# Two vector instructions moved ahead of three others in the first group of three MLP blocks

## The reference

```
xn = (x - mu) / sqrt(var + 1e-6) * g_ln
ch = max(xn @ w_ch1, 0) @ w_ch2        # 512 -> 2048 -> 512, 4 x 576 rows
x  = x + ch
```

## Time and profile before

| | |
|---|---|
| median of 3 runs | 932.4 us (932.03 to 933.45) |
| profiled execution | 932.03 us, span 930.2 us |
| PE busy / PEld busy | 908.8 us (98%) / 841.2 us (90%) |
| DVE / ACT / POOL busy | 707.1 us (76%) / 545.5 us (59%) / 552.2 us (59%) |
| first MLP, blocks 2, 3, 4 | about 444.5 to 710 us of the span |
| group 0 of blocks 2, 3, 4 | second products from 452.7, 539.2 and 625.9 us |

### The profile page before, as it was taken

The page is one execution under the profiler, slowest core; times in us unless marked ns, Lnnn a source line. Parts: engine busy times, 40 slices in busy tenths (PEclk is TensorE's granted clock), DMA queues, the critical chain, the costliest instruction groups (busy, mean ns, idle before and its releaser), DMA issues.

```text
span 930.2 us, 18185 instructions
## 1 busy us (share of the span) xinstructions
PE 908.8 (98%) x6153; PEld 841.2 (90%) x6153; DVE 707.1 (76%) x1155; ACT 545.5 (59%) x1184; POOL 552.2 (59%) x547
## 2 busy tenths in 40 slices
PE   4999999999999999999999999999999999999998
PEld 3999999999989999999899988898988989989897
DVE  4899989989998899942767878789998672663623
ACT  3899999999989666543655655565565221212110
POOL 4989889898873477665566668758986210010100
PEclk9999999999999999999999999999999999999999
DMA  6243233234213233100000000002200001010011
GB/s 179 65 104 93 68 94 100 66 90 103 69 41 110 71 95 122 35 1 1 1 1 1 1 1 1 1 3 68 91 25 1 1 1 46 1 50 8 1 47 57
DMA packets 44874, 44.46 MB, mean 48 GB/s; under 512 B 14017, under 2 KB 34753, under 8 KB 44673
## 3 DMA queue, kind: packets, MB, share of 16 engines
q1 hardware_dynamic: 44368, 43.21, 16.8%
q10 hardware_dynamic: 432, 0.30, 0.1%
HBM read 28.81 MB, written 4.72 MB: 36 GB/s over the span
## 4 chain that ended last, share of the span: by engine, by line
PE 87%; DVE 9%; ACT 2%; issue 1%; DMA 1%; SPq 0%; ACTq 0%; DVEq 0%
PE fc_ps L2132 16%; PE seven_ps L2162 14%; PE ring_ps L2028 8%; PE scores_ps L1964 7%; PE wide_ps L2331 6%; PE ring_ps L1975 6%; PE bank_ps L2287 5%; PE wide_ps L2310 5%; PE bank_ps L2345 5%; PE seven_ps L2212 2%; PE scores_ps L1957 2%; DVE lefts L1639 2%; PE seven_ps L2132 2%; DVE hid_sums L1627 2%; PE ring_ps L1911 2%
## 5 line engine op out<-in xcount | busy, mean ns | idle before, releaser
L2132 PE MATMUL fc_ps<-xT,W1s 128*128 128x512 f32 (+1 forms) x828 | 191.1, 379 | 0.4 <-ACT hid L1147 0.3
L2162 PE MATMUL seven_ps<-rights,lefts 128*128 128x256 f32 x1344 | 173.6, 284 | 0.0
L2162 PEld LDWEIGHTS seven_ps<-rights,lefts 128*128 128x128 f32 x1344 | 169.5, 191 | 4.4
L2132 PEld LDWEIGHTS fc_ps<-xT,W1s 128*128 128x128 f32 x828 | 146.2, 189 | 27.8 <-ACT hid L1147 1.3
L1453 DVE TENSOR_REDUCE nmax<-scores_ps 128x1 f32<-128x576 f32 x144 | 106.9, 753 | 17.0 <-PE scores_ps L1964 11.7
L946 POOL TENSOR_TENSOR rights<-w_rest,rights 128x256 fp32r<-128x256 f32 x84 | 81.6, 972 | 54.6 <-ACT rights L1190 54.6
L1053 ACT ACTIVATE E<-scores_ps,nmax 128x576 f32<-128x576 f32 x128 | 95.7, 749 | 10.7 <-DVE nmax L1453 9.8
L1462 DVE TENSOR_TENSOR prob_lo<-ring_ps,prob_hi 128x512 fp32r<-128x512 f32 x144 | 95.5, 683 | 2.1 <-ACT prob_hi L1067 1.7
L1008 POOL TENSOR_TENSOR rstd<-ve,power 128x1 f32<-128x1 f32 x18 | 14.5, 807 | 138.7 <-DVE ve L1821 138.7
L1067 ACT ACTIVATE prob_hi<-ring_ps 128x512 fp32r<-128x512 f32 x144 | 85.6, 613 | 4.3 <-PE ring_ps L1975 2.9
L1964 PE MATMUL scores_ps<-stack 128*128 128x288 f32 x256 | 81.4, 333 | 1.2 <-DMA swapped_k<-stack 0.8
(11 more groups left out here) (185 smaller groups left out, 2114.5 us busy)
## 6 DMA issues: line engine op xcount, KB each, us to landing
swapped_k<-stack SPq DMA_DIRECT2D x64, 144.0 KB, 2.5
w_raw<-in_w SPq DMA_DIRECT2D x18, 256.0 KB, 3.0
qk_raw<-in_k SPq DMA_DIRECT2D x16, 256.0 KB, 2.8
v_raw<-in_v SPq DMA_DIRECT2D x16, 256.0 KB, 2.8
qk_raw<-in_q SPq DMA_DIRECT2D x15, 256.0 KB, 2.8
w_rest<-in_w SPq DMA_DIRECT2D x7, 512.0 KB, 4.2
out<-out_sb SPq DMA_DIRECT2D x14, 256.0 KB, 2.4
w_raw<-in_win SPq DMA_DIRECT2D x4, 512.0 KB, 3.5
```

Of the source, the lines that this page charges most:

```text
L2132: mm = nc.tensor.matmul(fc1_bank(n, f)[:, 0:cols], W1s[:, slot1(f), w, c, :], xT[:, x, c, 0:cols], start=first, stop=(c == DC - 1 and x == 1))
L2162: mm = nc.tensor.matmul(seven_ps[k][:, 2 * P * a:2 * P * (a + 1)], lefts[:, k, x, P * a:P * (a + 1)], rights[:, k, w, :], start=(g == 0 an ...
```

## The change

In group 0 of the blocks 2, 3 and 4, DVE makes part 2 of the left low parts and the low parts of the right sums before the sums S1, S2 and S4, not after them. All other groups, and block 0, keep their order. Waits and instructions are otherwise the same.

```
@@ factors(n, g), vector block
                 if n == 2 and g == 0:
                     for t in range(2):
                         fold_tails(t)
+                if n > 0 and g == 0:
+                    left_low(n, g, 2)
+                    right_low_sums(n, g)
                 hid_sum(n, g, S1)
                 hid_sum(n, g, S2)
                 hid_sum(n, g, S4)
                 if last:
                     next_low(n, 0)
                     left_low(n, g, 1)
-                left_low(n, g, 2)
-                if n > 0 and g == 0:
-                    right_low_sums(n, g)
+                if n == 0 or g > 0:
+                    left_low(n, g, 2)
                 if n == 0 and g == 0:
                     merge_tails((2, 3))
                     right_low_sums(0, 0)
```

## The result

| | before | after |
|---|---|---|
| median of 5 runs each | 933.36 us | 938.63 us (937.14 to 940.23) |
| ratio | | 1.0059, 95% interval 1.0043 to 1.0076 |
| a second set (21 and 5 runs) | 932.85 us | 939.42 us (938.24 to 939.63), ratio 1.0068 (1.0054 to 1.0082) |
| profiled execution | 932.03 us, span 930.2 us | 939.09 us, span 937.3 us |
| PE / DVE busy | 908.8 / 707.1 us | 909.4 / 700.8 us |

What follows compares the result with a forecast made beforehand. PE, busy 98% of the span, was taken as the bound. Delays of 2.13 + 1.85 + 2.12 = 6.1 us in blocks 2 to 4 gave 938.1 us profiled, median 938.5 us; range 935.5 to 940.5.

Steps and rivals of the forecast that it cites:

- PE does not wait for any of these: Group 0, blocks 2 to 4: products 2 and 3 and POOL's weight sums get earlier, PE waits for none; gain 0.
- The chain S4, left high part 4, relu, hidden chunk: Group 0, blocks 2 to 4: later S4 delays left high part 4, the relu of f = 2, then hidden chunk f = 3.
- DVE's idle time ahead of left low part 2: Group 0, blocks 2 to 4: DVE stands idle some 0.7 to 1.1 us until ACT's high part 2 ends.
- S1 short, S2 and S4 long: Group 0: S1 as alone, next 0.46 us later; S2 and S4 beside POOL, 0.85 us each; 0.86 us per block.
- The rival without contention: Rival 2: S2 and S4 run as if alone, only the small cost, 3.5 us, 935.9 us; chance 0.15.
- PE late by 2.13, 1.85 and 2.67 us: Hidden chunk's weight loads in group 0 of blocks 2, 3 and 4 start that much later, waiting for the relu.
- What comes back in block 4: Later waits for DVE at the end of block 4 shrink by 0.55 us, so 2.12 of 2.67 us stays.
- DVE's shift of 2.12 us: Block 4: winS on DVE starts at 630.31 and not 628.19 us, so DVE's chain is 2.12 us later.
- Rival 1: Slack hides the move: no cost, or at most 0.75 us gained in block 4, 931.6 to 932.4 us; chance 0.05.
- The clock rival: Three stalls of about 2 us each drop PE's clock to half speed, 5.6 us more each, 955 us; chance 0.02.
- left low part 2 has slack to spare: 380 to 760 us: no row has the second products waiting for a low part, so making it earlier gains 0.

Runs made afterwards that it cites:

- the swapped order: Both instructions moved as in the changed kernel, but right low sums first and left low part 2 behind them; median +5.9 us (1.0061), stretch +7.69 us against the kernel before.

## Why the prediction was right

- "PE does not wait for any of these", so "the gain here is 0": right for products 2 and 3. Moving left low part 2 alone gave only a loss. For POOL's weight sums it was not quite right, as the point on block 4 below shows.
- The chain S4, left high part 4, relu, hidden chunk: shown, by the rows of the changed kernel and by putting the relu ahead, which takes 3.2 of the 5.3 us away with DVE's order unchanged.
- DVE's idle time ahead of left low part 2: forecast to start 0.03 us behind ACT; 541.28 + 0.63 to 541.95 is 0.04.
- S1 short, S2 and S4 long: 0.42, 0.84, 0.84 us. The rival without contention (3.5 us) is out; with POOL held back the cost was +2.85 us.
- PE late by 2.13, 1.85 and 2.67 us: measured 2.00, 1.72 and 2.66. In blocks 2 and 3 the relu followed a little closer on left high part 4: the relu ended 1.21 us behind S4's end (546.81 against 545.60, before 1.35).
- What comes back in block 4, the mis-sized term: 0.55 us forecast, 1.03 measured (2.66 of lateness, +1.63 in the stretch). I had carried DVE's shift of 2.12 us through the block unchanged. The first winS piece did start 2.09 us later against the block's second hidden chunk, but it took 1.21 us where it took 1.76. All engines, the kernel before, then the one after:

```profile
628.95 1.60 POOL L908 TENSOR_TENSOR w_sums<-w_rest,w_sums 128x256 f32<-128x256 f32 x1
```

```profile
634.52 0.79 POOL L910 TENSOR_TENSOR w_sums<-w_sums,w_rest 128x256 f32<-128x256 f32 x1
635.78 1.21 DVE L1773 TENSOR_TENSOR winS<-w_raw,winS 128x1024 fp32r<-128x1024 f32 x1
```

  Before, POOL was in the middle of its weight sums when the piece began at 628.19; now the last of them ends at 635.31, ahead of it. It is not PE's lateness that does this: the piece took 1.21 to 1.23 us in all seven profiles in which block 4 has the right low sums ahead and POOL is not held back (with the relu ahead PE was only 0.31 us late), 1.44 in the two with POOL held back, and 1.75 or 1.76 in all five with the right low sums at their old place. Rival 1 had named this effect ("shortens DVE in block 4"), and the sum left it out. The run with the relu ahead, read so, has DVE's chain 1.13 us later at the end of the block, not 2.12. In the changed kernel PE is later than that by its own wait, so both late waits go away: 0.90 us is back at the last hidden chunk, and another 0.12 ahead of the second MLP. What share the shorter DVE instructions behind the winS piece have was not taken apart. The sum is therefore 5.3 and not 6.1 us.
- The clock rival: I gave it 0.02, at 5.6 us a place and at all three. It was real at a smaller size: 1.6 us a fall. It came with block 4 alone in four of five runs by their mean clock; in the changed kernel one profile of two has it, at one place of three, and how often it comes there is open. The reason that I gave against it, a full clock in all 40 slices of the page, was a poor one: a slice is 23 us and its digit is cut at 9. The page of the swapped order, with two falls and a mean clock of 0.996, shows a 9 in every slice too. The Trainium skill says in "TensorE: Matmul & The Clock Gate" (Part 1) that the clock is gated down after idleness. The traces agree (waits of 2.06, 2.10, 2.59 and 4.02 us had a fall), though not each time (two other profiles with a wait of 2.59 us had none), so this rival should have had a higher chance.

So the mechanism was right, and the forecast of 938.5 us lies this close under the two medians of 938.63 and 939.42 partly by luck. 0.8 us too much waiting stood in for a clock loss of 0 to 1.6 us a profile that was left out; and the kernel before came out at 933.36 in that set, 0.96 above the 932.4 from which the forecast was added up. One more of its steps was too simple: that left low part 2 has slack to spare. When only the right low sums were moved, it was what PE waited for first.

## What to carry to other kernels

Before moving an instruction up in a queue, list what is queued behind those that it pushes down, on the other engines too, down to an instruction that needs none of them: here a relu behind a copy, and a PSUM bank behind the relu. An instruction moved ahead of a wait turns the wait into idle time of its engine; and what it releases on POOL can double the time of the DVE instructions that now run beside it, and shorten later ones that POOL no longer meets. Where PE has been dense, price each new wait with what the clock may do behind it, and look at the granted clock in stretches of a few microseconds, not in slices of the whole span.

## What the runs showed of the hardware

- The granted clock of PE fell from 2.4 to 1.2 GHz at one wait of 2.06, 2.10 or 2.59 us in a stream that was dense ahead of it, and was back within 4.2 us of work. It did so in one profile of the changed kernel and not in the other, with the same wait to 0.01 us. At waits of 1.92 us and less no profile showed it. At 4.02 us the profile shows it, back only after about 6 us of work, and the mean clock of all five runs is 0.996 or 0.997.
- Twelve weight loads for matmuls of 512 columns took 4.14 to 4.16 us and not 2.6 where the lower clock fell mostly on them; the loss for one such fall was 1.6 us, and 2.7 for the longer one.
- Two-input DVE instructions of 128x256 took 0.84 to 0.85 us beside POOL's and 0.42 alone, and holding POOL back alone switched between the two. In these rows it mattered which starts first: S1, 0.16 us ahead of POOL, took 0.42 us, and 0.32 us behind it (only the right low sums moved), 0.71.
